# One load in place of two: both halves of kv of batch 1 in a single transfer of 18432 bytes a row

## The reference

```python
kv = np.einsum('bhsd,bhse->bhde', k, v)
out = np.einsum('bhsd,bhde->bhse', q, kv)
rms = np.sqrt(np.mean(out * out, axis=-1, keepdims=True) + 1e-06)
x = out / rms * g_norm                    # as 4608 tokens x 512
logits = x @ phi                          # 32 slots, 4 for each of 8 experts
d = softmax of logits over the tokens;  slot_input = d.T @ x
h = np.maximum(slot_input[e] @ w1[e], 0);  slot_out[e] = h @ w2[e]
c = softmax of logits over the slots;   result = c @ slot_out
```

## Time and profile before

| | us |
|---|---|
| median of 3 runs | 171.94 |
| profiled execution | 172.04 |
| its span | 170.7 |
| TensorE (PE) busy | 151.3, 89% |
| VectorE busy | 86.6, 51% |
| ScalarE busy | 89.0, 52% |
| GpSimd busy | 59.6, 35% |
| SyncE's DMA queue, share of the 16 DMA engines | 97.8% |
| moved | 71.65 MB, 420 GB/s over the span |

### The profile page before, as it was taken

The page is one execution under the profiler, slowest core; times in us unless marked ns, Lnnn a source line. Parts: engine busy times, 40 slices in busy tenths (PEclk is TensorE's granted clock), DMA queues, the critical chain, the costliest instruction groups (busy, mean ns, idle before and its releaser), DMA issues.

```text
span 170.7 us, 4234 instructions
## 1 busy us (share of the span) xinstructions
PE 151.3 (89%) x1832; PEld 105.5 (62%) x1832; DVE 86.6 (51%) x185; ACT 89.0 (52%) x230; POOL 59.6 (35%) x73
## 2 busy tenths in 40 slices
PE   7989697989999899999899998989999989998700
PEld 3469576979778878897697674346665543345300
DVE  1122156284677266762946698823888137205700
ACT  3036576796975886859759864202223045205700
POOL 7000707638357745377382679500000004000000
PEclk9999999999999999999999999999999999699965
DMA  5999999999999999999999999999999999999988
GB/s 190 414 429 423 443 418 440 465 422 454 449 418 434 431 428 430 418 409 449 422 434 422 434 407 426 443 428 420 430 426 438 451 418 407 420 432 410 405 380 369
DMA packets 4365, 71.65 MB, mean 420 GB/s; under 512 B 790, under 2 KB 790, under 8 KB 922
## 3 DMA queue, kind: packets, MB, share of 16 engines
q1 hardware_dynamic: 3994, 71.18, 97.8%
q0 software_dynamic: 352, 0.20, 0.4%
HBM read 61.94 MB, written 9.44 MB: 418 GB/s over the span
## 4 chain that ended last, share of the span: by engine, by line
PE 59%; DMA 13%; ACT 12%; DVE 7%; SPq 2%; issue 1%
PE psum L214 59%; DMA arena<-in_kv_dram 13%; ACT bd L214 3%; ACT sq L214 3%; ACT xall L214 2%; SPq L214 2%; DVE arena L214 1%; DVE logits L214 1%; ACT arena L214 1%; DVE ms L214 1%; ACT part L214 1%; ACT d L214 1%; DVE part L214 1%; ACT r L214 1%; DVE acc L214 1%
## 5 line engine op out<-in xcount | busy, mean ns | idle before, releaser
L214 PE MATMUL psum<-bd,arena 128*128 128x192 f32 (+1 forms) x320 | 56.1, 335 | 1.9 <-ACT bd L214 1.5
L214 PEld LDWEIGHTS psum<-bd,arena 128*128 128x128 f32 (+1 forms) x320 | 45.4, 179 | 8.6 <-ACT bd L214 2.8
L214 DVE TENSOR_REDUCE ms<-sq 128x16 f32<-128x1024 f32 (+1 forms) x19 | 22.1, 1163 | 32.5 <-ACT sq L214 32.3
L214 POOL TENSOR_TENSOR part<-part,r 128x512 f32<-128x512 f32 x17 | 17.8, 1048 | 49.7 <-DVE r L214 49.7
L214 POOL TENSOR_TENSOR xall<-xall,r 128x512 f32<-128x512 f32 x34 | 34.7, 1042 | 0.0
L214 ACT ACTIVATE sq<-psum 128x512 f32<-128x512 f32 x36 | 21.5, 598 | 11.6 <-PE psum L214 11.3
L214 PEld LDWEIGHTS psum<-arena 128*64 128x64 f32 (+1 forms) x640 | 19.0, 137 | 8.3 <-DMA arena<-in_kv_dram 3.2
L214 PE MATMUL psum<-arena 128*64 128x64 f32 (+1 forms) x640 | 21.7, 226 | 2.2 <-DMA arena<-in_kv_dram 2.2
L214 ACT COPY xall<-psum 128x512 f32<-128x512 f32 x34 | 20.6, 606 | 0.0
L214 ACT COPY part<-psum 128x256 f32<-128x256 f32 (+1 forms) x38 | 13.6, 359 | 12.9 <-DVE part L214 11.7
L214 DVE TENSOR_REDUCE logits<-part 128x64 f32<-128x512 f32 (+1 forms) x18 | 17.8, 990 | 0.0
(11 more groups left out here) (80 smaller groups left out, 124.8 us busy)
## 6 DMA issues: line engine op xcount, KB each, us to landing
arena<-in_w_dram SPq DMA_DIRECT2D x4, 4096.0 KB, 23.5
arena<-in_w_dram SPq DMA_DIRECT2D x4, 2048.0 KB, 20.0
arena<-in_t_dram SPq DMA_DIRECT2D x1, 6912.0 KB, 36.0
arena<-in_w_dram SPq DMA_DIRECT2D x2, 3072.0 KB, 22.7
arena<-in_kv_dram SPq DMA_DIRECT2D x2, 2304.0 KB, 23.5
arena<-in_kv_dram SPq DMA_DIRECT2D x1, 4608.0 KB, 42.6
arena<-in_kv_dram SPq DMA_DIRECT2D x1, 3584.0 KB, 32.1
arena<-in_kv_dram SPq DMA_DIRECT2D x3, 1152.0 KB, 12.0
```

The lines of the kernel that those rows point to most:

```text
L214: inst = getattr(engine, method)(*args, **kwargs)
```

## The change

The two transfers of batch 1's kv, 9216 bytes a row each, become one of 18432 bytes a row, into the same place of `arena`. The bytes are the same, and so is the order of the transfers around it.

```diff
     load_row(Q_AT[0], q0_in[:, :2048])
-    load_row(KV_AT[1], kv_in[1, :, :2304])
-    load_row(KV_AT[1] + 9, kv_in[1, :, 2304:])
+    load_row(KV_AT[1], kv_in[1])
     load_row(Q_AT[0] + 8, q0_in[:, 2048:])
     load_row(KV_AT[2], kv_in[2])
```

## The result

The changed kernel takes 172.84 us (median of 20 runs, 171.81 to 175.65); the kernel before, beside it on the same chip, 171.93 us (20 runs, 171.79 to 172.22). The ratio is 1.005 with a 95% interval of 1.0029 to 1.0071; it leaves out executions more than 1.5% above the fastest, while the two medians are over all 20. So it is slower by about 0.9 us; forecast were 173.2 and a range of 171.9 to 174.2. But the spread is new: 0.4 us became 3.8 us. And the times of the changed kernel don't fill that spread evenly. They lie in three groups: 171.8 to 172.1 (5 runs), 172.4 to 173.4 (7) and 174.0 to 175.7 (8). The execution that was profiled is the fastest, 171.81 us with a span of 170.5, which is no slower than before. A reader who has only this profile would find no loss in it.

The account below looks back on a forecast made before the run. Data bounds the kernel until 26.9 us, then compute with TensorE. Late start 3.64, less 1.06 (old wait and slack before step 1) and 1.33 (wait before batch 2), gives 1.25: 171.94 + 1.25 = 173.2 us, range 171.9 to 174.2.

Parts of the forecast that it names:

- The late start and its way through TensorE: Step 0 of batch 1 starts 3.64 us later; tiles follow, the old wait swallows 1.33, step 0 of batch 2 +1.25.
- computing behind it neither absorbs nor adds: Behind step 0 of batch 2 no load is waited for; ScalarE at tile 6 costs 0, at most 0.4 us.
- The length of the rows: Longer rows in the merged transfer of batch 1: costed at 0, at most 0.1 us either way.
- the one issue less on SyncE: SyncE issues one instruction less, some 0.44 us; later transfers wait in the queue anyway, so it brings nothing.
- the fetch: An instruction block fetched at 15.1 us through the same DMA engines makes batch 1's landing 1.5 us later, at 18.4.
- Rival 1: Instruction fetch held back while TensorE waits for batch 1; landing at 16.9, no cost, 171.9 us; chance 0.13.
- rival 4: The 1.5 us are the second transfer's own cost and go with it; landing at 16.9, 171.9 us; chance 0.04.
- So the whole 1.25 us arrives at the end.: At the last stores the queue has run dry, so the delay passes fully to the end: 1.25 us, bounds 0 and 1.25.
- rival 2: TensorE's clock falls to half in the wait for batch 1: 174.2 us, or 175.5 if down through tile 4; chance 0.11.
- a small rival: Less arrives at the end, by where the half clock of 146.67 to 150.08 falls or a shorter gap: 172.5 us; chance 0.08.

Follow-up runs that it names:

- experiment 5: The kernel before without the 2048 KB load of w1 of expert 7: median 170.19 us, ratio 0.9917 to the whole kernel before.
- experiment 7: The changed kernel with 14 matmuls on zeros in its wait and without the load of w1 of expert 7: 171.38 us, ratio 0.9978 to the whole kernel before.
- experiment 2: The kernel before, still with two transfers for batch 1, but the second half loaded ahead of the first: 172.87 us, ratio 1.0074.
- experiment 8: The changed kernel a third time, no edit, one execution: 173.84 us.
- experiment 1: The changed kernel run again, no edit: 172.79 us, ratio 1.0092; the profiled execution took 171.84.
- experiment 3: The changed kernel with 14 matmuls on zeros in front of step 0 of batch 1, keeping TensorE busy in the wait: 171.87 us, ratio 1.0003.
- experiment 4: The changed kernel with step 0 of batch 1 moved behind the products of tile 2: 171.88 us, ratio 1.0013.
- experiment 6: The changed kernel without the 2048 KB load of w1 of expert 7: 174.25 us, ratio 1.0049 to the whole kernel before.

## Why the prediction was right in size, by luck, and wrong in its end

**Right.** The late start and its way through TensorE: each start came 0.27 us earlier than forecast, because the transfer landed 0.27 earlier (18.11, forecast 18.38), and the distances 1.08 and 1.50 us held exactly. Forecast 18.43, 19.51, 21.01, 28.17; measured 18.16, 19.24, 20.74, 27.90. The delay at step 0 of batch 2 was 0.98 us for a forecast of 1.25. That computing behind it neither absorbs nor adds is shown by experiments 5 and 7 (1.26 us there, 1.24 us at the last issue). The length of the rows and the one issue less on SyncE were worth nothing, as costed (experiment 2).

**Right, with more to it: the fetch.** Rival 1 was wrong: the fetch isn't held back by the wait. In the profile of the result it comes before the wait begins, at 13.4 to 13.6:

```profile
q8 instruction: 1, 0.02, 29.0%
```

In experiments 2 and 8 it comes at 15.1 and 14.7, 0.5 and 0.3 us behind the moment at which TensorE stopped. Experiment 5, a kernel whose first loads are those of before, had its first fetch at 13.4 to 13.6 too, and there the first half of batch 1 takes 13.4 us to land instead of 12.0 (the fetch, then the landing):

```profile
q8 instruction: 1, 0.02, 30.0%
...
arena<-in_kv_dram SPq DMA_DIRECT2D x1, 1152.0 KB, 13.4
```

So the transfer under way when the fetch comes lands 1.4 us later. The second half, with no fetch in its way, landed at 18.1 there, 2.6 us behind the first; before, with the fetch between the two, it was 4.3 us. The 1.5 us that I had put down to the fetch are its own, and rival 4 (a cost of a second transfer) falls with this. Nor did joining bring the landing forward by more than executions differ: the last of batch 1 lands at 18.1 to 18.4 in the three profiles with two transfers, at 17.9 to 18.3 in the seven with one. The Trainium skill gives a fixed cost of about 2.0 us a DMA ("DMA: Bandwidth & Descriptors", "Anatomy of one DMA"). It gives it for transfers issued from GpSimd, while these are issued from SyncE, and its remark on two halves ("Rules for kernel authors") is on halves of the partitions, while these are halves of each row. Between the two transfers of experiment 5 no such cost is to be seen.

**Wrong: "So the whole 1.25 us arrives at the end."** This step failed. I read from one stretch in which the DMA engines were at 0.78 that the queue had run dry and that stores go when computed. That held in that execution, since it had its own fall of the clock late in the kernel, 1.9 us, which had eaten the slack. In the profiles with no fall of the clock before the last store (the result's and experiments 1, 3 and 4) the queue is the bound, with a span of 170.5 to 170.7, and 1.6 to 1.7 us of late computing cost nothing. The clock at half from 146.67 to 150.08 stood in my own rows; I used it for a small rival and not for the question of what the end would be without it. My bounds for this step were 0 and 1.25. With the full clock it is 0 for a delay of 0.9 to 1.0 us.

**Wrong: the weight of rival 2.** The fall of the clock had a chance of 0.11. No loss is left without it: hold TensorE busy and the ratio is 1.0003 (experiment 3). With it the delay counts as well, since the two share the 1.7 us that the queue hides: without the 1.0 us of delay the execution of experiment 8 would have ended at 171.5 instead of 172.5 (an estimate from its own profile). The times that the rival gave, 174.2 and 175.5, lie in the third group, but not by its sum: it added 1.0 and 2.3 us to 173.2. Measured against the result's profile, the fall made step 0 of batch 2 start 1.49 us later in experiment 6 and 2.65 in experiment 8, on a time of 171.8, and the queue hid 0.7 of it; 175.5 needs a late fall on top. I held against the rival that the work just before the stop was dense. In three of the five profiles with a stop of 3.3 to 3.8 us the clock fell all the same: 0.51 of the clock over 6.3 us behind a wait of 3.61 in experiment 8. The Trainium skill warns of waits for a DMA between bursts of matmuls ("TensorE: Matmul & The Clock Gate", "HAM oscillation"); these three profiles agree with it, and the other two kept the full clock.

**The groups put together.** The end is the later of two: 170.5, and the last issue plus 8.7. The last issue is the start of step 0 of batch 2 plus 133.2, and 1.7 to 1.9 more with a late fall of the clock. The time is 1.3 more than the span.

| | step 0 of batch 2 | last issue | plus 8.7 | time |
|---|---|---|---|---|
| delay, full clock | 27.90 | 161.1 | 169.8, below 170.5 | 171.8 |
| delay, fall as in experiment 6 | 29.39 | 162.6 | 171.3 | 172.6 |
| delay, fall as in experiment 8 | 30.55 | 163.8 | 172.5 | 173.8 |
| the same and a late fall | 30.55 | 165.5 | 174.2 | 175.5 |

The second row fits the second group. So would the delay with a late fall alone, 161.1 + 1.7 + 8.7 = 171.5 and a time near 172.8: its mean clock would be about the same, and no execution of the second group with the load in place was profiled. It can't be frequent, for of the 23 executions of experiments 3 and 7, which keep the clock in the wait, only one (172.81) is where a late fall would put it. So the median of 172.84 lies in the second group and is near 173.2 by luck: the forecast let a delay of 1.25 us through to the end at the full clock, where none of it arrives, and what makes the median later is the clock, which it had left to a rival.

**Open.** Whether the clock falls isn't decided by the kernel: the same program kept it (experiment 1's profile) and lost it (experiment 8's). The waits of the profiles that kept it were 3.28 and 3.43 us, of those that lost it 3.52, 3.61 and 3.82; five profiles are too few to make a limit of that. Nor did the clock fall at the same place: at 17.4 us (experiment 8) and 17.9 (2), inside the wait, and at 19.4 (6), 1.4 us behind it. What differs between two executions was not found. I didn't find a version faster than both; experiments 3 and 4 come back to the time of before and no further, which fits a bound by the DMA queue.

## What to carry to other kernels

Joining two transfers moves the first consumer from the landing of its part to the landing of the last byte; look at what stands between the two consumers. When TensorE is made to wait for several us, price the clock behind the wait as well as the delay, and keep the engine busy if the wait must stay. Before a delay is passed on to the end, compute both ends, that of the work and that of the queue, and make sure that the profiled execution isn't one with a disturbance of its own there: a kernel with two bounds close together hides up to their distance and nothing beyond.

## What the runs showed of the hardware

- A wait of 3.3 to 3.8 us on TensorE brought half the clock for over 3 us (experiment 6) or over 6 us (2, 8) in three profiles of five, and not in the other two (the first profile and experiment 1). With 14 matmuls on zeros in the wait it stayed at full there in both profiles (experiments 3 and 7).
- A fall of some 3.4 us late in the kernel moved the last issue back by 1.9 us (before) and 1.7 us (experiment 6), against 133.2 us from step 0 of batch 2 in the eight other profiles.
- At half the clock the products of a tile (128x192) took 2.93 us for 1.57, and the kv products (128x64) 1.98 for 1.15.
- With the fetch of one block of instructions, 0.02 MB, in its way a transfer of 1152 KB landed 1.4 us later (13.4 us in experiment 5, 12.0 before). The fetch came at 15.1 us in one of these and at 13.5 in the other, though both begin with the same instructions.
